# Attention in units of 64 rows by 96 keys, two units on the halves of the partitions

## The reference

```python
scores = scale * np.matmul(q, k.transpose(0, 1, 3, 2))
rel = pos[:, None] - pos[None, :]
mask_local = (rel >= 0) & (rel < stride)                     # stride = 32
mask_strided = (rel >= 0) & (pos[None, :] % stride == pos[:, None] % stride)
scores = np.where(masks[None, :, :, :], scores, -1000000000.0)
scores = scores - np.max(scores, axis=-1, keepdims=True)
attn = np.exp(scores)
attn = attn / (np.sum(attn, axis=-1, keepdims=True) + 1e-09)
return np.matmul(attn, v).astype(np.float32)
```

## Time and profile before

| | |
|---|---|
| three runs | 591.85, 592.8 and 593.96 us, median 592.8 |
| the profiled execution | 592.75 us, its span 591.0 us |
| PE busy | 576.5 us, 98% of the span |
| chain that ended last | 94% PE |
| slices 1 to 8 of 40 (14.8 us each) | attention; PE 8 or 9 tenths busy, DVE and ACT 6 to 8, DMA 6 to 9 |
| granted TensorE clock | 0.995 of full speed as a mean |

### The profile page before, as it was taken

How to read it: one execution, slowest core, us unless ns; L and a number is a source line. 1 busy time by engine, 2 the same in 40 slices (tenths; PEclk the granted TensorE clock), 3 DMA queues, 4 the chain that set the end, 5 groups by cost and what they waited for, 6 DMA issues and landing times.

```text
span 591.0 us, 10967 instructions
## 1 busy us (share of the span) xinstructions
PE 576.5 (98%) x3609; PEld 460.2 (78%) x3610; DVE 299.0 (51%) x690; ACT 227.3 (38%) x709; POOL 145.1 (25%) x170
## 2 busy tenths in 40 slices
PE   8999999999999999999999999998999999999995
PEld 4777777768887888888888878997989545888883
DVE  4888888686665866566665613358112112220200
ACT  4888988742333333434434322211122201221210
POOL 6776767530100001422233000010001111011011
PEclk9999999999999999999999999999999999999999
DMA  9777678100000160000000000000951370001001
GB/s 196 180 172 198 172 179 186 49 1 19 36 18 19 65 256 18 35 18 18 18 21 33 18 19 1 34 36 27 406 189 35 124 239 25 1 19 51 1 24 43
DMA packets 68878, 47.24 MB, mean 80 GB/s; under 512 B 54744, under 2 KB 56760, under 8 KB 68848
## 3 DMA queue, kind: packets, MB, share of 16 engines
q1 hardware_dynamic: 64560, 40.49, 23.7%
q0 software_dynamic: 1920, 5.77, 2.7%
q10 hardware_dynamic: 2368, 0.59, 0.6%
HBM read 37.40 MB, written 9.96 MB: 80 GB/s over the span
## 4 chain that ended last, share of the span: by engine, by line
PE 94%; DVE 2%; DMA 2%; issue 1%; ACT 0%; ACTq 0%; POOL 0%; POOLq 0%; DVEq 0%
PE pair L616 17%; PE bank L616 17%; PE pair L1031 10%; PE bank L1046 9%; PE bank L1157 7%; PE pair L1145 6%; PE pair L753 5%; PE bank L781 4%; PE bank L764 4%; PE pair L735 4%; PE pair L1231 3%; PE pair L1824 2%; PE pair L1802 2%; PE pair L749 2%; PE bank L1251 1%; DMA arena<-in_k 1%
## 5 line engine op out<-in xcount | busy, mean ns | idle before, releaser
L616 PE MATMUL pair<-w_hi,wide_x 128*128 128x512 f32 x288 | 98.1, 399 | 0.0
L616 PE MATMUL bank<-w_hi,wide_x 128*128 128x512 f32 x288 | 92.0, 390 | 0.0
L616 PEld LDWEIGHTS bank<-w_hi,wide_x 128*128 128x128 f32 x288 | 54.0, 188 | 12.9 <-issue 1.7
L1102 POOL DMA_INDIRECT out<-work,lead_sidx x18 | 18.0, 1002 | 186.9 <-ACT work L1201 79.7
L616 PEld LDWEIGHTS pair<-w_hi,wide_x 128*128 128x128 f32 x288 | 54.1, 188 | 11.2 <-issue 0.3
L1701 POOL TENSOR_TENSOR rstd<-ln_small 128x1 f32 (+1 forms) x18 | 16.8, 931 | 175.0 <-DVE ln_small L684 175.0
L1031 PE MATMUL pair<-wide_x,lead_hi 128*128 128x256 f32 x320 | 58.2, 284 | 0.0
L616 PE MATMUL pair<-w_lo,wide_x 128*128 128x512 f32 x144 | 56.1, 389 | 0.0
L616 PE MATMUL bank<-w_lo,wide_x 128*128 128x512 f32 x144 | 56.0, 389 | 0.0
L1031 PEld LDWEIGHTS pair<-wide_x,lead_hi 128*128 128x128 f32 x320 | 50.1, 192 | 0.3
L1031 PE MATMUL pair<-wide_x,lead_lo 128*128 128x256 f32 x160 | 45.3, 283 | 0.0
(11 more groups left out here) (245 smaller groups left out, 1149.0 us busy)
## 6 DMA issues: line engine op xcount, KB each, us to landing
entry<-in_moe_w SPq DMA_DIRECT2D x12, 1024.0 KB, 9.3
arena<-in_q SPq DMA_DIRECT2D x32, 144.0 KB, 2.8
x_dram<-work SPq DMA_DIRECT2D x18, 256.0 KB, 2.0
arena<-in_moe_w SPq DMA_DIRECT2D x8, 512.0 KB, 7.5
arena<-in_k SPq DMA_DIRECT2D x28, 144.0 KB, 3.1
arena<-in_v SPq DMA_DIRECT2D x16, 144.0 KB, 2.3
work<-in_v SPq DMA_DIRECT2D x16, 135.0 KB
arena<-in_moe_w_in SPq DMA_DIRECT2D x8, 256.0 KB, 3.1
```

The costliest lines, as they stand in the source:

```text
L616: ins = pe.matmul(ps[:, cols], a, b, start=first and n == 1, stop=last and n == 3 * len(lhs))
```

## The change

Local heads are cut into 9 units (`NU`) of 64 rows by 96 keys (`UR`, `UK`). Strided heads are cut into 11 units, ten of three residues (54 rows by 54 keys) and one of two (36 by 36). Two units of the same head lie on partitions 0 to 63 and 64 to 127 of one block of scores, so a group of four units has four blocks (two for each head) of 128 rows; the last local group has one unit, whose two heads share one block. A score matmul has 64 rows of the array (the head) and 64 columns (the unit's half). Strided values take their keys from the partitions of their head (v of head 1 is loaded to partitions 64 and up), local ones as before from 0. Strided probabilities lie side by side, 64 columns for each head, so that one transpose of 128 by 128 turns four of them. Everything else of the program stays. The diff, cut to its core:

```diff
-    ST = 5
+    ST = 11
-    GROUPS = [(True, [0, 1]), (True, [2, 3]), (True, [4, 5]), (False, [0, 1]), (False, [2, 3]), (False, [4])]
+    UR = P // 2
+    UK = UR + STRIDE
+    NU = S // UR
+    GROUPS = [(True, [(0, 1), (2, 3)]), (True, [(4, 5), (6, 7)]), (True, [(8,)]),
+              (False, [(0, 1), (2, 3)]), (False, [(4, 5), (6, 7)]), (False, [(8, 9), (10,)])]
...
-        mask_local0 = sb("mask_local0", HALF, BF16)
-        mask_local = sb("mask_local", HALF, BF16)
-        mask_strided = sb("mask_strided", 4 * SR, BF16)
+        mask_local = sb("mask_local", 2 * UK, BF16)
+        mask_strided = sb("mask_strided", SR, BF16)
...
+        def members(g):
+            local, blocks = GROUPS[g]
+            if packed(g):
+                return [(0, hh, blocks[0][0], hh) for hh in range(2)]
+            return [(n, hh, t, half) for n, units in enumerate(blocks) for half, t in enumerate(units) for hh in range(2)]
...
              def load_v(i, kind):
...
+                        blocks = heads[bass.ds(lead + hh, 1)].rearrange("o (j p) d -> p (o j) d", j=NU)
+                        sp.dma_start(dst[STRIDE:UK, hh, :, :], blocks).then_inc(ld_v[0], 16)
+                        sp.dma_start(dst[0:STRIDE, hh, 1:NU, :], blocks[UR - STRIDE:UR, 0:NU - 1]).then_inc(ld_v[0], 16)
...
-                        dst = v_str[:, hh * ST * D:(hh + 1) * ST * D]
+                        dst = v_str[hh * UR:hh * UR + SR, :]
                         src = heads[bass.ds(lead + hh, 1)].rearrange("o (a r) d -> (o a) (r d)", r=STRIDE)
                         main = src[:, 0:RMIN * ST * D].rearrange("a (s n) -> s a n", s=RMIN)
                         sp.dma_start(dst[0:RMIN * NA, :], main).then_inc(ld_v[1], 16)
...
             def scores(i, g):
-                for hh in range(2):
-                    pe.matmul(score_cols(g, hh, 0, len(tiles)), ident_bf[0:rows, 0:rows], mask_of(g), start=True, stop=False)
-                for n, t in enumerate(tiles):
-                    for hh in range(2):
-                        part = slice(hh * D, (hh + 1) * D)
-                        ins = pe.matmul(score_cols(g, hh, n), q_cols(local, t)[part], k_cols(local, t)[part],
-                                        start=False, stop=(t == tiles[-1]))
+                for hh in range(1 if packed(g) else 2):
+                    pe.matmul(score_cols(g, hh, 0, len(blocks)), ident_bf[:, :], mask_of(g), start=True, stop=True)
+                for n, hh, t, half in members(g):
+                    part = slice(hh * D, (hh + 1) * D)
+                    rows = slice(half * UR, half * UR + unit_rows(local, t))
+                    ins = pe.matmul(score_cols(g, hh, n)[rows, 0:unit_keys(local, t)], q_cols(local, t)[part],
+                                    k_cols(local, t)[part], start=False, stop=True, skip_group_check=True)
...
             def turn_probs(i, g):
-                for n in range(2 * len(tiles)):
-                    ins = pe.transpose(pT_ps[0:keys, n * rows:(n + 1) * rows],
-                                       probs[g % 3][0:rows, n * keys:(n + 1) * keys], ident[0:rows, 0:rows])
+                width = UK if local else P
+                for n in range(n_blocks(g) if local else len(blocks)):
+                    ins = pe.transpose(pT_ps[0:width, n * P:(n + 1) * P],
+                                       probs[g % 3][:, n * width:(n + 1) * width], ident[:, :])
...
             def values(i, g):
+                if not local and not static(i):
+                    pause(pe)
+                for n, hh, t, half in members(g):
+                    rows, keys = unit_rows(local, t), unit_keys(local, t)
+                    at_ = (block_of(g, n, hh) if local else n) * P + half * UR
+                    key0 = 0 if local else hh * UR
+                    to = 0 if packed(g) else (2 * n + half) * (UR if local else SR)
+                    ins = pe.matmul(o_ps[hh * D:(hh + 1) * D, to:to + rows], v_tile(local, t, hh),
+                                    probs_T[g % 2][key0:key0 + keys, at_:at_ + rows],
+                                    start=True, stop=True, skip_group_check=True)
...
             def exps(i, g):
+                for n in range(len(GROUPS[g][1])):
+                    for hh in range(1 if packed(g) else 2):
+                        b = block_of(g, n, hh)
+                        ins = act.activation(probs[g % 3][:, b * width:b * width + keys], score_cols(g, hh, n),
+                                             ACT.Exp, bias=neg_max[g % 2][:, b:b + 1],
+                                             accum_out=row_sum[g % 3][:, b:b + 1])
...
             def take_o(i, g):
...
+                both = span[:, 0:RMIN * ST, :].rearrange("p (s t) a -> p t s a", s=RMIN)
+                act.copy(both[:, first:first + len(units)], src[:, :, 0:RMIN, :])
+                ins = act.copy(span[:, RMIN * ST + first:RMIN * ST + first + whole, :], src[:, 0:whole, RMIN, :])
...
+            dve.memset(probs[2], 0.0)
```

More of the change, by code:

```diff
@@ new lines, in attention_pool @@
+            for base, rows in ((UR, P), (0, UR)):
+                part = local[0:rows]
+                link(pool.memset(part, 0.0))
+                link(pool.affine_select(out=part, in_=part, compare_op=ALU.is_ge, fill=MASKED, base=base - 1,
+                                        pattern=[[0, 2], [1, UK]], channel_multiplier=-1))
+                link(pool.affine_select(out=part, in_=part, compare_op=ALU.is_ge, fill=MASKED, base=STRIDE - base,
+                                        pattern=[[0, 2], [-1, UK]], channel_multiplier=1))
@@ L551, in attention_pool @@
+            last.then_inc(mask_ready, 1)
             pool.memset(ones_bf[:, :], 1.0)
@@ L824, in exps @@
             def exps(i, g):
-                local, tiles = GROUPS[g]
-                rows, keys = rows_keys(g)
+                keys, width = keys_of(g), width_of(g)
                 c = NG * i + g
@@ L848, in take_o @@
                     return
                 span = xT[:, bass.ds(token0 + 2 * T, S)].rearrange("p (a r) -> p r a", r=STRIDE)
-                for n, t in enumerate(tiles):
-                    ins = act.copy(span[:, t:STRIDE:ST, :],
-                                   src[:, n * rows:(n + 1) * rows].rearrange("p (r a) -> p r a", a=NA))
+                src = o_ps[:, 0:len(units) * SR].rearrange("p (t s a) -> p t s a", t=len(units), s=RMAX)
+                first, whole = units[0], sum(RES[t] == RMAX for t in units)
```

156 lines of the change are left out of this document (70 added, 86 removed).

## The result

The changed kernel takes 632.0 us (median of four runs, 631.8 to 633.1) against 593.3 us in the same comparison for the kernel before: a ratio of 1.066, 95% interval 1.0635 to 1.0685. It is slower by 38.7 us where 9 us less were forecast. The profiled execution took 633.1 us, its span is 631.3 us, 40.3 above before's.

A forecast was written before the change was run, and what follows sets the result against it. PE bounds the kernel at 13.19 us a round; after the change SP paces at 12.05, above PE's 11.55. Six rounds save 6.8 us, round 0 1.0, round 7 1.4: 9.2 off 592.75 gives 583.5 us, range 579.5 to 590.5.

The forecast's parts named there:

- PE's price of the new work: PE's attention round: scores, masks and probability transposes gain 1.10, 0.43 and 0.32 us, values lose 0.21; 13.19 to 11.55 us.
- rival 2: Scores: array quarters overlap only in pairs, so score steps double; PE 12.6 us a round, 588 us; chance 0.09.
- rival 3: Strided values and last local scores: two row halves writing one bank take turns; PE 12.9 us, 590.3 us; chance 0.10.
- rival 4: Scores and values: PE can't start records faster than 40 ns; a round of 14.5 us, slower at 603 us; chance 0.08.
- the estimate of 12.25 us from the Trainium skill: PE's round if starts never come closer than about 25 ns: 0.40 us for a full score group's steps, some 585 us.
- PE is busy for all of it at full granted clock: Steady attention, 20 to 90 us: PE busy throughout at full clock, so PE sets the pace, ACT close behind with 89%.
- The last sentence of the prediction: A granted clock below 1.00 in the first 120 us would break every step; given no chance.
- Only the strided v change: SP's queue: of its transfers only strided v changes form, taking 0.45 us off 12.5 and leaving 12.05 us a round.
- rival 1: SP keeps 0.79 us for a strided v main issue; the round is 12.5 us, the time 586.2 us; chance 0.15.
- my 0.55: SP's strided v main issues of 36 runs: 0.55 us each taken, between bounds of 0.32 and 0.79.
- The reserve it first eats is small: K's landing at 78.1 us before its transposes at 79.92: 1.8 us reserve, less 1.1 by which slots between get shorter.
- 2.4 forecast for round 0 and the tail: Gain outside the six steady rounds: 1.0 us in round 0 and 1.4 us in round 7 with its tail.

The follow-up runs named there:

- e17: Changed kernel issuing no Q, K or V loads in rounds 1 to 5, eight 512-column matmuls ahead of each round 1 waiting place; 606.3 us, other tokens later.
- e8: Changed kernel with every score matmul on all 128 array rows instead of 64, leaving out the heads' separation in the scores; 600.4 us, ratio 1.0142.
- e1: Changed kernel with eight 512-column matmuls ahead of each of the two instructions where PE stood still in round 1; 622.2 us, ratio 1.0515.
- e14: Changed kernel with three 512-column matmuls ahead of both waiting places in rounds 1 to 6, constants' loads behind strided V; 599.3 us, ratio 1.006.
- e4: Changed kernel with two 512-column matmuls ahead of the values in each slot of rounds 1 to 6; 601.6 us, ratio 1.0178.
- e7: Changed kernel with ten 512-column matmuls in one place, ahead of the values in the second slot of round 3; 623.3 us, ratio 1.0509.
- e10: Changed kernel with V's loads of rounds 1 to 5 cut to one row (or one a block); executions 608.5, 622.0, 647.5, 647.6 us.
- e11: Changed kernel with the next round's two weight loads issued by POOL behind its rounding instead of by SP; 628.6 us, ratio 1.0607.
- e11b: Changed kernel with the next round's two weight loads issued by ACT in the third slot instead of by SP; 628.5 us, ratio 1.0643.
- e15: Changed kernel with one-row Q, K and V loads in rounds 1 to 5 and sixteen 512-column matmuls in round 1; 638.1 us, one execution, other tokens later.
- e12: Changed kernel with three 512-column matmuls ahead of both waiting places in rounds 1 to 6, constants' loads behind strided V, weight loads on POOL; 602.2 us, ratio 1.017.
- e6: Changed kernel with one 512-column matmul ahead of the values in each slot of rounds 1 to 6; 606.9 us, ratio 1.0227.
- e9: Kernel before with 20 semaphore instructions on PE's queue at each of two places of round 1; 600.7 us, ratio 1.0181.

## Why the prediction was wrong, point by point

- **PE's price of the new work: right, where the clock is full.** 11.55 us a round were forecast, 11.71 measured in e17. Local scores 0.49 (0.48), strided ones 0.35 (0.35), strided values 0.61 (0.58). The 0.49 for 16 records against e8's 0.86 on half as many tiles shows that the quarters do run four at a time. Rivals 2, 3 and 4 fall, and so does the estimate of 12.25 us from the Trainium skill (TensorE: Matmul & The Clock Gate, "Wait — 56ns, not 53.3ns?"): a full group of strided scores took 0.35 us here, where that estimate has 0.40 for its 16 records alone.
- **"PE is busy for all of it at full granted clock": the step that failed.** This was a true reading of the kernel before. Every duration in the sum came from a row at 1.00, and the sum took for granted that the new work would be run at 1.00 too. The last sentence of the prediction said that a lower clock would break every step; no case and no chance stood for it. The runs showed instead that the clock falls to 0.50 at the first long waits and that this work doesn't bring it back: 19.72 us a round in the changed kernel, for the same instructions that take 11.71 at 1.00 in e17, with PE never idle in either.
- **"Only the strided v change": the second.** Local V's transfers changed form too, from 6 blocks to 9, which costs SP 0.97 us a round. Strided main issues measured 0.72 and 0.68 us, nearer to rival 1's 0.79 than to my 0.55, so strided V gave back some 0.2 us and not 0.45. The issues of K behind it took 1.78 us in e1, 0.8 more than in most rounds of before. 12.5 + 0.97 - 0.2 + 0.8 is 14.1 us, which is e1's measured 14.08 and not 12.05.
- **"The reserve it first eats is small" was right, and its consequence was missed.** 0.5 us a round of waiting was costed as 0.5 us. The waits came unevenly instead, 0.3 to 3.2 us at one place, and some of those of 1.1 us and more are paid a second time, in clock.
- **How much each failure cost.** With the clock kept, six rounds at 14.1 us instead of 13.19 lose 5.5 us, against 2.4 forecast for round 0 and the tail: some 596 us, estimated; no run has the changed kernel's full work and loads at 1.00 throughout. e14's best executions (593.2 to 596.7 us), with their six stirs a round, lie there. So by this estimate the supply alone turned the 9 us gain into a small loss, and the clock turned that into 39 us. A slower outcome had only rival 4, on a ground that doesn't hold.

The Trainium skill (TensorE: Matmul & The Clock Gate, "HAM oscillation — how this bites in real kernels") describes a kernel whose waits for DMA, some 3 to 5 us each, drop the clock again and again, and names more or wider work between waits as the cure. The traces agree that waits for DMA drop the clock, here with shorter ones (1.60 and 1.64 us), and that wider work helps (e4). They differ on the way back: there each busy stretch warms the array again, here PE was busy 10.00 of 10 us for 120 us at 0.50.

What stays open. Whether scores on quarters alone do it, or only together with the transposes and narrow values around them, was not separated: e8 changed the scores, and no run changed the others. In e8 the scores also take longer (0.86 us for 0.49), so their larger share of the time was not told apart from their rows. What decides whether a given gap drops the clock is open too. Nor was a version tried that fills the whole array's rows and keeps the heads apart, for instance with zeros in the other head's half of q.

## What to carry to other kernels

Before work is cut into smaller tiles of the array, ask whether the new work could win the full clock back after one late load; a row of the old kernel at full clock says nothing about that. Then compute the supply at the shorter round, with each transfer whose shape changes, since a compute engine that just passes its feeder turns a hidden wait into a gap. Where gaps can't be closed, wide matmuls put ahead of the waiting instruction can keep the clock at the price of their own time: two in each slot, 2.6 us a round, took 30 us off this kernel, which still stayed 1.8% slower than the one before.

## What the runs showed of the hardware that I had not expected

- The changed kernel has a half-clock stretch of 122 us (28 to 151 us) with PE busy in nearly all of it. In e7 ten 512-column matmuls ended such a stretch within 3 us, and in e8 one of 10 us was ended by score matmuls with as few columns but twice the rows.
- The same quarter-sized work keeps 1.00 for 76 us when it is never kept waiting (e17). Holding the clock and winning it back are different questions.
- Whether a gap drops the clock is not decided by its length alone. With the changed kernel's work and no stirs beside it, 1.18 us (e10), 1.34 us (e11) and 1.63 us (e11b) didn't drop it at once; 1.10 us (e7), 1.20 us (e15) and 1.64 us (e1) did, within 2 us. With two stirs a slot 1.37 us didn't (e4), with three ahead of the wait 2.01 us didn't (e14) and 1.39 us did (e12); with one a slot 1.20 us did (e6). In the old kernel 1.66 us didn't in the profiled execution (e9).
- The time that SP needs to issue a transfer doesn't go by its bytes: 0.33 us for 6 blocks of 96 rows, 0.70 for 9 of 64, and 0.84 for 9 blocks of one row (e10). One form isn't always one price either: two issues of K took 1.00 to 2.82 us in e14.
- Semaphore instructions on PE's queue cost 0.15 us each once the first nine or so are spent, which don't show as a gap: at the first place 14 made a gap of 0.73 us, 20 one of 1.66 and 50 one of 6.22.
